# Linear attention and two expert stages on one core: the first unit's key sums as 36 one-column products on TensorE, with GpSimd's list of work put in another order

## The reference, cut to what matters

```python
def phi(x):
    proj = np.einsum('bhsd,df->bhsf', x, w_phi)
    proj = proj - np.max(np.abs(proj), axis=-1, keepdims=True)
    return np.concatenate([np.exp(proj), np.exp(-proj)], axis=-1)
q_p, k_p = (phi(q), phi(k))
kv = np.einsum('bhsf,bhsd->bhfd', k_p, v)
z = np.sum(k_p, axis=2)
num = np.einsum('bhsf,bhfd->bhsd', q_p, kv)
den = np.einsum('bhsf,bhf->bhs', q_p, z)[..., None] + 1e-06
return (num / den).astype(np.float32)
```

## Time and profile before

| | |
|---|---|
| time, median of 3 runs | 854.54 us (852.8 to 854.9) |
| the profiled execution | 854.62 us |
| its span, first to last instruction | 852.8 us |
| TensorE busy | 836.7 us, 98% |
| VectorE, ScalarE, GpSimd busy | 47%, 40%, 29% |
| attention on TensorE | from 1.5 us to about 170 us |

### The profile page before, as it was taken

The page is one execution under the profiler, slowest core; times in us unless marked ns, Lnnn a source line. Parts: engine busy times, 40 slices in busy tenths (PEclk is TensorE's granted clock), DMA queues, the critical chain, the costliest instruction groups (busy, mean ns, idle before and its releaser), DMA issues.

```text
span 852.8 us, 19744 instructions
## 1 busy us (share of the span) xinstructions
PE 836.7 (98%) x7380; PEld 724.5 (85%) x7381; DVE 401.9 (47%) x731; ACT 339.0 (40%) x752; POOL 244.7 (29%) x288
## 2 busy tenths in 40 slices
PE   8999999999999999999999999999999999999996
PEld 6898999799999899789989998988778888888885
DVE  4677777511155345325535763552774522512221
ACT  4677677411046226314613622551342423422221
POOL 4977887794000000000000000019252122112211
PEclk9999999999999999999999999999999999999999
DMA  6544343239432012102101210513432611311111
GB/s 159 141 138 127 108 121 95 62 124 26 1 87 63 25 50 62 38 1 75 63 13 50 65 34 38 198 50 122 175 102 97 241 49 50 117 48 49 44 34 48
DMA packets 36174, 68.03 MB, mean 80 GB/s; under 512 B 11352, under 2 KB 11480, under 8 KB 36120
## 3 DMA queue, kind: packets, MB, share of 16 engines
q1 hardware_dynamic: 26168, 44.90, 20.4%
q10 hardware_dynamic: 6512, 11.64, 4.8%
q0 software_dynamic: 3440, 10.75, 3.9%
HBM read 57.84 MB, written 9.98 MB: 80 GB/s over the span
## 4 chain that ended last, share of the span: by engine, by line
PE 92%; DVE 2%; POOL 2%; ACT 2%; issue 1%; ACTq 0%; POOLq 0%; DVEq 0%
PE bank L1747 24%; PE bank L1749 23%; PE bank L1748 23%; PE bank L1687 4%; PE bank L1632 4%; PE bank L1657 4%; PE bank L1642 1%; PE bank L1958 1%; PE bank L1794 1%; PE bank L1620 1%; PE bank L1823 1%; PE bank L1673 1%; DVE stage L1210 1%; ACT stage L1013 1%; PE bank L1950 1%
## 5 line engine op out<-in xcount | busy, mean ns | idle before, releaser
L1179 DVE SCALAR_TENSOR_TENSOR hid_lo<-bank,hid_hi 128x384 fp32r<-128x384 f32 x96 | 53.5, 558 | 209.1 <-ACT hid_hi L989 209.1
L1749 PE MATMUL bank<-uT_hi,W 128*128 128x384 f32 x384 | 129.6, 337 | 0.0
L1747 PE MATMUL bank<-uT_hi,W 128*128 128x384 f32 x384 | 129.4, 337 | 0.0
L1748 PE MATMUL bank<-uT_lo,W 128*128 128x384 f32 x384 | 128.9, 336 | 0.0
L989 ACT ACTIVATE hid_hi<-bank 128x384 fp32r<-128x384 f32 x96 | 46.9, 488 | 186.1 <-PE bank L1749 178.8
L1013 ACT ACTIVATE stage<-stage 128x512 f32<-128x512 f32 x135 | 84.6, 627 | 78.2 <-DVE stage L1210 71.7
L1747 PE MATMUL bank<-W,hid_hi 128*128 128x512 f32 x288 | 114.0, 396 | 0.3 <-DVE hid_lo L1179 0.3
L1749 PE MATMUL bank<-W,hid_lo 128*128 128x512 f32 x288 | 113.7, 395 | 0.0
L1748 PE MATMUL bank<-W,hid_hi 128*128 128x512 f32 x288 | 113.4, 394 | 0.0
L1210 DVE TENSOR_TENSOR stage<-rows,stage 128x512 f32<-128x512 f32 x135 | 89.0, 687 | 11.8 <-ACT stage L1013 8.5
L1448 DVE TENSOR_TENSOR hT_lo<-bank,hT_hi 128x512 fp32r<-128x512 f32 x34 | 23.4, 687 | 130.5 <-ACT hT_hi L1076 130.1
(11 more groups left out here) (305 smaller groups left out, 1535.5 us busy)
## 6 DMA issues: line engine op xcount, KB each, us to landing
rows<-in_moe_w SPq DMA_DIRECT2D x12, 1024.0 KB, 6.3
stage<-gate_rows ACTq DMA_DIRECT2D x38, 256.0 KB, 3.2
stage<-in_moe_w_ch SPq DMA_DIRECT2D x16, 512.0 KB, 4.3
qk_raw<-in_q SPq DMA_DIRECT2D x32, 144.0 KB, 3.7
vv<-in_v SPq DMA_DIRECT2D x32, 144.0 KB, 2.8
x_rows<-rows SPq DMA_DIRECT2D x6, 768.0 KB, 3.3
qk_raw<-in_k SPq DMA_DIRECT2D x30, 144.0 KB, 3.7
late_stage<-in_moe_w SPq DMA_DIRECT2D x4, 1024.0 KB, 6.8
```

The costliest lines, as they stand in the source:

```text
L1179: dve.scalar_tensor_tensor(out=hid_lo[:, n % 2], in0=bank[:, HB[n % 2], 0:TOK], scalar=0.0, in1=hid_hi[:, n % 2].bitcast(F32), op0=ALU.max ...
L1747: pe.matmul(dst, lhs_hi, rhs_hi, start=start, stop=False)
L1748: pe.matmul(dst, lhs_hi, rhs_lo, start=False, stop=False)
L1749: return pe.matmul(dst, lhs_lo, rhs_hi, start=False, stop=stop)
```

## The change

Three things are changed. In step 2 alone, TensorE no longer waits for GpSimd's key sums but makes unit 0's itself: for each of the two signs, nine tiles and two halves, a product with a tile of `kp` as the stationary operand and one column of ones as the moving one, summed in PSUM (36 products in place of 4). GpSimd drops `sum_keys(0)`, places and rounds V without a break, then waits for TensorE's first `kv_summed` and counts `k_summed` up itself. And both subtractions of V (`rest_of_v(0)` and `rest_of_v(1)`), one of which stood ahead of `sum_keys(1)` and one behind it, now stand behind `sum_keys(1)`.

```diff
             def sum_keys(u):
-                par, old = u % 2, KSTEPS * u
-                if u > 0:
-                    pool.wait_ge(k_summed, u)
+                par, old = u % 2, KSTEPS * (u - 1)
+                pool.wait_ge(k_summed, u)
...
             for n in range(3):
                 place_v(n)
-            sum_keys(0)
-            pool.wait_ge(k_summed, 1)
             place_v(3)
             round_v()
-            rest_of_v(0)
+            pool.wait_ge(kv_summed, 1)
+            pool.sem_inc(k_summed, 1)
             sum_keys(1)
             pool.wait_ge(k_summed, 2)
+            rest_of_v(0)
             rest_of_v(1)
...
-                    pe.wait_ge(k_summed, u + 1)
-                    settled(pe)
-                    for sign in range(2):
-                        for half, rr in enumerate(HALVES):
-                            mm = pe.matmul(bank[:, KV_BANK + half, K_SUMS.start + sign:K_SUMS.start + sign + 1],
-                                           k_sum[par][rr, sign, :], ones[rr, 0:1], start=True, stop=True)
+                    if is_step(s, 2):
+                        for sign in range(2):
+                            for t in range(T):
+                                for half, rr in enumerate(HALVES):
+                                    mm = pe.matmul(bank[:, KV_BANK + half, K_SUMS.start + sign:K_SUMS.start + sign + 1],
+                                                   kp[par][rr, t // GT, t % GT, sign, :], ones[rr, 0:1],
+                                                   start=(t == 0), stop=(t == T - 1))
+                    else:
+                        pe.wait_ge(k_summed, u + 1)
+                        settled(pe)
+                        for sign in range(2):
+                            for half, rr in enumerate(HALVES):
+                                mm = pe.matmul(bank[:, KV_BANK + half, K_SUMS.start + sign:K_SUMS.start + sign + 1],
+                                               k_sum[par][rr, sign, :], ones[rr, 0:1], start=True, stop=True)
                     mm.then_inc(kv_summed, 1)
```

## The result

The changed kernel took 859.79 us (median of 5 runs, 859.11 to 861.02) against 854.54 us (852.8 to 854.91): ratio 1.0069, interval 1.0057 to 1.0080. It is 5.3 us slower. The profiled execution took 860.41 us with a span of 858.2.

The account below looks back on a forecast made before the run. TensorE, busy 836.7 of 852.8 us, was taken to carry any early delay to the end. Unit 2's products 3.4 us later plus 1.27 for a second half-clock stretch made 4.7: 859.3, median 859.2 us, range 856.6 to 861.3.

Parts of the forecast that it names:

- The spacing of the products: Step 2: 72 records start 0.052 us apart, with five in the half-clock stretch adding 0.3 us in all.
- products at the half clock: Rival, chance 0.12: clock falls in the middle of step 2's products, 20 records cost 1.4 us more; 860.6, up to 862.
- cheap products: Rival, chance 0.08: each one-column product in step 2 costs 0.03 us; 856.4 us, or 857.7 with a fall in step 4.
- the half-clock stretch behind step 2: Clock falls at 24.17 us until about 27.58, costing output products 0.77 us instead of 1.27; step 3 starts 1.9 later.
- the products hold the clock: Rival, chance 0.12: 36 products without a gap keep 2.4 GHz in step 2, so its half-clock stretch goes; 856.9 us.
- Unit 1's sums: Step 3: GpSimd's adds hang on ScalarE's third key group; TensorE's wait of 0.44 us shrinks to about 0.2.
- Unit 2's sums: Step 4: behind two subtractions they end at 45.45 us; TensorE waits 1.9 us, its products start 3.4 us later.
- The clock in step 4: A second half-clock stretch behind the new wait in step 4, six in ten, costing 1.27 us.

Follow-up runs that it names:

- twelve products: Kernel before with late subtractions, step 2 using twelve products on three partial sums instead of four, GpSimd making six adds for unit 0: 853.04 us against 853.87.
- products alone: Changed kernel with both subtractions of V moved into GpSimd's idle stretch ahead of its wait for the first `kv_summed`: 856.86 us against 854.21.
- wider products: Changed kernel with 28 columns of ones instead of one in each of the 36 products: 859.54 us against 854.21.
- The fill: Kernel before with four unread products of 122 columns on TensorE ahead of its step 2 wait for unit 0's key sums: 854.08 us against 854.21.
- order alone: Kernel before with both subtractions of V behind `sum_keys(1)`, unit 0's key sums staying on GpSimd: 855.40 us against 854.21.
- late subtractions: Kernel before with both subtractions of V moved behind the key sums of unit 14: 853.95 us against 853.87.

## Why the prediction was right

The time (859.79 against 859.2), the direction and the two causes were right: the products in step 2 and the order of GpSimd's list each cost time by themselves. The sizes inside were less so.

1. **The spacing of the products was right, their sum was too small.** At the full clock, 24 records ran 0.052 us apart in the run with twelve products. Between 19.69 and 22.8 us the 72 also kept near it (57 records started, 0.055 apart). But the clock fell at about 22.9 and not behind their end. From first start to last it took 4.92 - 0.35 = 4.57 us (0.35 us is the longest record, at the half clock), where I had 3.98 with the last five slowed. I had this as a rival, "products at the half clock", at 0.12; it is what the traces of the changed kernel, of the products alone and of the wider products all show. The rival "cheap products" leaned on 25 ns from the Trainium skill, "TensorE: Matmul & The Clock Gate", section "Back-to-back issue gap". That section gives the figure for matmuls taken by themselves and says that in a stream with loads of the stationary operand both set the spacing, so my row of 0.052 us and the Trainium skill do not disagree, other than the prediction says.

2. **The step that failed is the half-clock stretch behind step 2.** I let it end where it ended before, with 0.77 us lost on the output products. It went on to 29.6 us: output products to the next transposes took 31.41 - 25.17 = 6.24 us against 4.26 at the full clock, 1.98 lost. Step 3 started 3.86 us late in the table, not 1.9; of the 2.0 us too little, 0.7 lie on the products of point 1 and 1.2 on the stretch behind them. The rival that the products hold the clock does not fit the three traces with the 36 products: in each the clock fell in the middle of 4.6 to 4.9 us of products without a gap. It is not refuted for every execution. Two of the changed kernel's five had a mean granted clock of 0.997 and 0.996, room for at most 6.0 and 7.7 us at the half clock, of which the end takes at least 1.6 in every trace here; the 6.6 us stretch cannot have come in them. They took 859.29 and 859.11 us, 1.2 less than the other three on average and far above that rival's 856.9. What held them up instead is not known, so the price of this stretch at the end of the execution is not settled by the traces.

3. **Unit 1's sums were as worked out.** GpSimd waited for ScalarE's third group, and the wait before the products is gone. The timeline of GpSimd:

```profile
32.21 0.73 POOL L792 TENSOR_TENSOR k_part<-kp 128x256 f32<-128x256 f32 x1 [2.72 <-ACT kp L944]
...
34.39 0.73 POOL L800 TENSOR_TENSOR k_sum<-k_part 128x256 f32<-128x256 f32 x1
35.19 5.35 POOL L776 TENSOR_TENSOR v_hl<-v_pair,v_hl 32x1152 fp32r<-32x1152 f32 x2
...
45.55 0.72 POOL L800 TENSOR_TENSOR k_sum<-k_part 128x256 f32<-128x256 f32 x1
```

4. **Unit 2's sums were right to 0.1 us.** From L792's start to unit 2's last add's end it is 46.27 - 32.21 = 14.06 us; the prediction's chain had 45.45 - 31.34 = 14.11. The wait was 1.83 us for 1.9. What I did not ask is where else the subtractions could stand: GpSimd was idle for 8.66 us up to 26.07, and the products alone show that in that gap they cost nothing.

5. **The clock in step 4** fell as forecast: 47.70 to 53.05, 5.35 us, against 4.22 in the same place before (43.28 to 47.50), 1.13 us for my 1.27.

6. **Why the total still came out.** By the table, 6.66 us were lost from the turn of the state on, against 4.7 forecast; that is the 2 us of point 2 too little. The medians differ by 5.3. The turn of unit 0's state itself came 1.1 us earlier in the trace of after, and two of its five executions had less half-clock time than the trace. Neither was forecast, and both bring the time nearer to my sum. So the close hit of the median is in part luck.

7. **What was wrong in the reading of before.** I priced its half-clock stretch at 1.27 us. The fill shows that without it step 3's key-sum products follow those of step 2 no sooner (10.93 us against 10.95), because GpSimd's chain ran beside it. In the trace of the changed kernel TensorE itself is on the path there, so there it is right to count the stretch.

The two halves add up: in step 5, 3.23 us for the products alone and 2.97 for the order alone make 6.20 of the 6.64 in the changed kernel; the 0.36 us won in step 3 is counted in both, which leaves 0.08. In the medians 2.65 and 1.2 make 3.9 of 5.3; some of that gap is the same 0.36, and the rest may lie with the executions of the order alone that had no fall of the clock in step 4; this is not shown.

## What to carry to other kernels

Moving a sum from a slow engine to TensorE costs by the number of stationary operands, not by the columns: 36 products here cost 4.6 us to fill a wait of 1.04, and twelve, which finish what the other engine has half done, cost 1.2 us and, together with the late subtractions, brought no loss that the times can show. When work is put behind a wait to clear the way for one unit, look at what then stands between this unit and the next, and whether the wait's own idle time would have held it. And before a stall or a slow stretch is priced, ask which other chain ends at the same place: here the half-clock stretch of step 2 and GpSimd's chain lay side by side, and taking away one or both moved the time by nothing that could be measured.

## What the runs showed of the hardware that I had not expected

A run of small products without a gap need not keep TensorE at 2.4 GHz: in the three traces with 72 such records, two of them with one column and one with 28, the granted clock fell to 0.50 in their middle and stayed there for 6.6 us or a little more, with TensorE and its weight loads busy nearly throughout (6.60 and 6.37 us of 6.60 in the changed kernel). In the two traces with 24 such records it did not fall. The same kernel can do both: two of five executions of the changed kernel had too little half-clock time for this stretch.

TensorE can stop for 0.5 to 1.6 us in the middle of a run of products with nothing shown that it waits for. The stops moved from step 3 to steps 4 and 5 when two large loads were moved, and those of 0.8 us and more came in or right behind a stretch of full DMA engines. In the kernel before with its weight pieces loaded later they came together with a loss of 1.1 us. What TensorE waits for in them is not shown.
